# One more pair with seven products, batch 1 transposed in fewer steps, and GpSimd's copy moved up: a fused attention, FFT and FFN kernel on one core

## The chip, the core and the metric

The kernel runs on one core of a Trainium2 chip. A core has TensorE (matrix products, into PSUM), VectorE, ScalarE, GpSimd and SyncE, which here only starts DMAs. In the profile they are PE (and PEld, the weight load), DVE, ACT, POOL and SP. Each runs its own list of instructions in order and meets the others through semaphores. The metric is the device time of one execution in microseconds.

## What is computed

Two batches, 768 rows, 512 columns. Attention in buckets gives x; then a two-dimensional Fourier transform (its real part), a normalised feed-forward network with a hidden width of 2048, and a gated output. The change touches the feed-forward network alone.

```python
def _moe_ref(x, w_ch1, w_ch2) -> np.ndarray:
    X = np.fft.fft(x, axis=1)
    X = np.fft.fft(X, axis=2)
    mixed = np.real(X).astype(np.float32)
    u = x + mixed
    mu = np.mean(u, axis=-1, keepdims=True)
    var = np.mean((u - mu) ** 2, axis=-1, keepdims=True)
    un = (u - mu) / np.sqrt(var + 1e-06)
    ch = np.maximum(un @ w_ch1, 0.0) @ w_ch2
    return (u + ch).astype(np.float32)

def _moe2_ref(x, w_val, conv_w, w_out) -> np.ndarray:
    B, S, D = x.shape
    K = conv_w.shape[0]
    xp = np.concatenate([np.zeros((B, K - 1, D), dtype=np.float32), x], axis=1)
    gate_pre = np.zeros((B, S, D), dtype=np.float32)
    for k in range(K):
        gate_pre += conv_w[k][None, None, :] * xp[:, k:k + S, :]
    gate = 1.0 / (1.0 + np.exp(-gate_pre))
    val = x @ w_val
    return (gate * val @ w_out).astype(np.float32)
```

## The kernel before

Every large product is made of three: each operand is split in a rounded high part (`_hi`, by ScalarE) and the rest (`_lo`, by VectorE or GpSimd), and hi x hi, lo x hi and hi x lo are added in PSUM.

The hidden width is 16 blocks of 128 for each batch, so 32 blocks in all. They are worked in two ways.

**Plain blocks** (`PLAIN` = 8 of batch 0). In step n TensorE does the first half of block n (`ffn1`: 24 matmuls from un to the hidden block, in two chunks of 512 and 256 columns in banks 6 and 7), then the second half of block n - 1 (`ffn2`: four pieces d of 6 matmuls into the accumulators). ScalarE takes the relu (`h_hi`), VectorE the rest (`h_lo`, `relu_lo`), which frees the bank. In `ffn2` of block n, before its piece d = 1, stands `transpose_un(T + n)`: tile n of batch 1 (T = 6 tiles of 128 rows) through bank 6, for n = 0 to 5; it waits until the first chunk of the next block has left bank 6. ScalarE and VectorE then make the tile's high part (`unT_hi`) and low part (`unT_lo`).

**Windows** (`WINDOWS` = 12, each one pair of blocks): the first half of a pair is done with seven products of half size instead of eight (Strassen's scheme), 42 matmuls of 384 columns, each product followed by one piece of the second half of the pair before it; an eighth piece closes the window. The operands of the products are sums: of w1, by GpSimd (`sum_w1_pair`, four additions, and `split_w1_pair`, seven low parts), and of un, by VectorE (`sum_un`, eight additions of 128x768 elements for each batch, and `split_unsum`, four low parts; ScalarE rounds in between with `round_unsum`). For batch 0 these are placed in plain steps 2 to 6; for batch 1 in windows 0 to 3. ScalarE copies the first product of a window out of PSUM (`copy_first`), and VectorE adds the others to it (`add_partial`); TensorE's third product waits for the first such sum.

**The seam** is window `SEAM` = 4, where batch 0 ends and batch 1 begins. In it the accumulators of batch 0 are completed; ScalarE and VectorE copy them out as x2 (`take_x2`), and GpSimd copies four columns at the border of each half for the convolution (`finish_x2`, L755), once all of x2 is there. VectorE (L1554) and ScalarE (L1144) both wait at the end of this window for that copy (`x2_lead` = 2). GpSimd's order in a window is: four low parts of the next pair's w1, low part of w2, the three other low parts of w1, four sums for the pair after that, low part of the other w2; in the seam `finish_x2` follows. Seven windows follow the seam, in which ScalarE and VectorE also do the convolution of batch 0 (`first_tap`, `conv_tap`).

SyncE starts the loads of weights in the order of their use. The load of the first pair of w1 (`load_w1_pair(0)`) waits for the end of the feature transform, since it goes to a place that the transform's tables share; it stands behind the loads of block 3.

## Time and profile before

| what | us |
|---|---|
| median of three runs | 625.12 (624.51 to 625.20) |
| the profiled execution | 624.13 |
| its span, first to last instruction | 622.5 |
| TensorE busy in it | 606.5 |
| VectorE, ScalarE, GpSimd busy | 427.0, 345.5, 342.0 |
| mean granted TensorE clock | 0.997 of full speed |

The plain steps run from about 282 to 346 us of the span, the windows from there to about 549, the output stage to the end. A row of a timeline gives start, duration, engine, line, operation, the tiles it writes and reads, and in brackets the idle time before it with what ended it. Durations of matmuls are longer than the distance of their starts, because they are pipelined: the distance of starts is what counts. The share of busy time is an average over stages; the waits and the stretches tell where an edit can act.

### The profile page before, as it was taken

How to read it: one execution, taken by the hardware profiler on the slowest of the kernel's cores; microseconds unless marked ns; L12 is line 12 of the kernel's file. 1: busy time of each engine (PE TensorE's matmuls, PEld its weight loads, DVE VectorE, ACT ScalarE, POOL GpSimd, SP SyncE). 2: the span in 40 equal slices, each digit the busy share in tenths (PEclk: the TensorE clock that was granted, in tenths of full speed). 3: DMA queues.
4: the chain of work that ended last, by engine and by line, in shares of the span. 5: the costliest groups of instructions: out<-in, count | busy, mean ns of one | idle time of the engine just before them, and what ended most of it. 6: DMA issues, size and time to landing. Idle time of an engine off the chain costs nothing.

```text
span 622.5 us, 10883 instructions
## 1 busy us (share of the span) xinstructions
PE 606.5 (97%) x3682; PEld 503.9 (81%) x3682; DVE 427.0 (69%) x683; ACT 345.5 (55%) x694; POOL 342.0 (55%) x328
## 2 busy tenths in 40 slices
PE   6899999999999999999999999997999999999997
PEld 3677777677777776998888999997899999988886
DVE  3978888888888875887465566635477666569920
ACT  4877777777777784464344444423444444274232
POOL 4543433333347664346335898865699999224140
PEclk9999999999999999999999999999899999999999
DMA  6942323323333020000312122230222222100102
GB/s 139 240 113 64 90 65 89 89 63 90 81 99 98 13 65 1 0 2 6 115 51 67 52 70 68 67 101 19 68 84 84 82 73 66 34 0 1 68 34 103
DMA packets 28178, 42.22 MB, mean 68 GB/s; under 512 B 3440, under 2 KB 16240, under 8 KB 28144
## 3 DMA queue, kind: packets, MB, share of 16 engines
q1 hardware_dynamic: 26176, 37.38, 21.1%
q0 software_dynamic: 1728, 4.02, 2.6%
q10 hardware_dynamic: 240, 0.39, 0.4%
q8 instruction: 18, 0.29, 0.2%
q14 instruction: 16, 0.13, 0.1%
HBM read 38.63 MB, written 3.15 MB: 67 GB/s over the span
## 4 chain that ended last, share of the span: by engine, by line
PE 93%; POOL 2%; DVE 2%; DMA 1%; issue 1%; ACT 1%; SPq 0%; ACTq 0%; DVEq 0%; POOLq 0%
PE banks L1876 21%; PE banks L1908 14%; PE banks L1663 12%; PE banks L1680 11%; PE banks L1730 10%; PE banks L1867 5%; PE banks L1990 5%; PE banks L2006 5%; PE banks L1703 2%; PE banks L1813 2%; PE banks L1616 2%; PE banks L1738 1%; DMA q_raw<-in_q 1%; PE banks L1622 1%; PE banks L1787 1%
## 5 line engine op out<-in xcount | busy, mean ns | idle before, releaser
L1242 DVE TENSOR_REDUCE row_min<-banks 128x1 f32<-128x768 f32 x96 | 91.8, 956 | 32.2 <-PE banks L1663 31.4
L872 ACT ACTIVATE prob<-banks,row_min 128x768 f32<-128x768 f32 x96 | 87.0, 906 | 29.0 <-DVE row_min L1242 28.9
L1730 PE MATMUL banks<-ident,prob 128*128 128x128 f32 x576 | 79.3, 273 | 1.4 <-ACT probT L374 1.4
L1502 DVE TENSOR_TENSOR partial_sums<-banks,partial_sums 128x384 f32<-128x384 f32 x72 | 40.1, 557 | 54.5 <-PE banks L1908 48.7
L1730 PEld LDWEIGHTS banks<-ident,prob 128*128 128x128 f32 x576 | 68.1, 140 | 6.8 <-issue 1.9
L1680 PE MATMUL banks<-probT,v_in 128*64 128x384 f32 x384 | 69.0, 494 | 0.0
L605 POOL TENSOR_TENSOR k_b<-k_raw,k_a 64x768 fp32r<-64x768 f32 x16 | 29.2, 1826 | 70.4 <-ACT k_a L855 70.3
L1876 PE MATMUL banks<-h_hi,w_hi 128*128 128x512 f32 (+1 forms) x256 | 66.4, 341 | 0.0
L1876 PE MATMUL banks<-h_hi,w_lo 128*128 128x512 f32 (+1 forms) x256 | 66.0, 339 | 0.0
L1876 PE MATMUL banks<-h_lo,w_hi 128*128 128x512 f32 (+1 forms) x256 | 65.7, 338 | 0.0
L374 ACT COPY probT<-banks 128x384 f32<-128x384 f32 x104 | 49.0, 479 | 22.5 <-PE banks L1730 22.2
L1663 PE MATMUL banks<-k_a,q_a 128*128 128x384 f32 x192 | 57.2, 379 | 2.6 <-POOL q_a L610 1.8
L1460 DVE SCALAR_TENSOR_TENSOR x_then_u_then_gate<-x2T,taps,x_then_u_then_gate 128x384 f32<-128x384 f32 x64 | 54.9, 862 | 3.9 <-ACT x_then_u_then_gate L1051 2.9
L1509 DVE SCALAR_TENSOR_TENSOR h_lo<-partial_sums,h_hi 128x384 fp32r<-128x384 f32 x48 | 43.0, 916 | 19.7 <-ACT h_hi L1098 19.7
L610 POOL TENSOR_TENSOR q_a<-q_raw,q_a 64x768 fp32r<-64x768 f32 x16 | 29.2, 1824 | 47.7 <-ACT q_a L859 47.5
L1663 PEld LDWEIGHTS banks<-k_a,q_a 128*128 128x128 f32 x192 | 29.5, 189 | 31.4 <-issue 28.5
L676 POOL TENSOR_TENSOR w_lo<-w_stage,w_hi 128x512 fp32r<-128x512 f32 x32 | 43.0, 1345 | 20.0 <-ACT w_hi L908 20.0
L374 DVE COPY probT<-banks 128x384 f32<-128x384 f32 x88 | 48.2, 548 | 2.8 <-PE banks L1730 2.8
L1663 PE MATMUL banks<-k_b,q_b 128*128 128x384 f32 x192 | 49.4, 338 | 0.0
L1680 PEld LDWEIGHTS banks<-probT,v_in 128*64 128x64 f32 x384 | 24.7, 136 | 28.6 <-issue 28.6
L1876 PEld LDWEIGHTS banks<-h_hi,w_hi 128*128 128x128 f32 x256 | 44.0, 189 | 1.5
L1876 PEld LDWEIGHTS banks<-h_lo,w_hi 128*128 128x128 f32 x256 | 39.4, 189 | 5.7
(216 smaller groups left out, 1497.4 us busy)
## 6 DMA issues: line engine op xcount, KB each, us to landing
w_stage<-in_moe_w_ch SPq DMA_DIRECT2D x40, 256.0 KB, 2.7
q_raw<-in_q SPq DMA_DIRECT2D x32, 192.0 KB, 3.3
k_raw<-in_k SPq DMA_DIRECT2D x30, 192.0 KB, 3.6
v_in<-in_v SPq DMA_DIRECT2D x16, 192.0 KB, 2.8
w_pair<-in_moe_w_ch SPq DMA_DIRECT2D x6, 512.0 KB, 3.8
w_stage<-in_moe_w_ch SPq DMA_DIRECT2D x6, 512.0 KB, 3.8
out<-y_out SPq DMA_DIRECT2D x11, 256.0 KB, 2.0
seq_tables_sb<-in_dft POOLq DMA_DIRECT2D x6, 386.0 KB, 3.5
```

The source lines that it names most:

```text
L374: copy(dst, src).then_inc(scratch_free[bank_of(i, use)], 1)
L676: pool.tensor_tensor(w2_lo[:, slot, :], w2_stage[:, slot, :], w2_hi[:, slot, :].bitcast(F32), ALU.subtract).then_inc(w2_lo_done, 1)
L872: act.activation(prob[s % 2][:, :, :], s_tile(s), ACT.Exp, bias=row_min[:, s:s + 1], scale=-1.0, accum_out=row_sum[:, s:s + 1]).then_inc(e ...
L1242: dve.tensor_reduce(row_min[:, s:s + 1], s_tile(s), AX.XY, ALU.min).then_inc(min_ready, 1)
L1460: dve.scalar_tensor_tensor(out=dst, in0=src, scalar=weight, in1=dst, op0=ALU.mult, op1=ALU.add).then_inc(conv_step, 1)
L1502: dve.tensor_tensor(out, product_bank[PRODUCT_BANK[o]], other, ALU.add).then_inc(done, 1)
L1509: dve.scalar_tensor_tensor(out=h_lo[:, slot, cols], in0=quarter[q], scalar=0.0, in1=h_hi[:, slot, cols].bitcast(F32), op0=ALU.max, op1=ALU ...
L1663: op = pe.matmul(s_tile(s)[:, c, :], lhs[:, rows], rhs[:, c * HALF:(c + 1) * HALF], start=start, stop=not start)
L1680: op = pe.matmul(PS[g * D:(g + 1) * D, 7, 0:HALF], v_in[:, h, kt, :], probT[h][:, kt, g * HALF:(g + 1) * HALF], start=(kt == 0), stop=(kt ...
L1730: op = pe.transpose(bank[:, j * P:(j + 1) * P], prob[tile % 2][:, c, j * P:(j + 1) * P], ident[:, :])
L1876: op = pe.matmul(acc(d, c), w_[:, m % 2 if isinstance(m, int) else 1 - slot, cols], h_[:, slot, at:at + size], start=False, stop=last, ski ...
L1908: op = pe.matmul(product_bank[PRODUCT_BANK[o]], w_[:, k, :], x_[:, k, :], start=OPENS_BANK[o] and k == 0 and n == 0, stop=(k == 1 and n == 2),
```

## The change

`PLAIN` goes from 8 to 6, so there are 13 windows instead of 12, five of them ahead of the seam (now window 5). The eight windows from the seam on stay. The six tiles of batch 1 are transposed in four steps: one in each of the second halves of blocks 0 and 1, two in each of blocks 2 and 3. The second tile of such a pair goes through bank 7 and waits for the second chunk's bank; the first half of the block after it waits for the first tile's low part with its first chunk and for the second tile's with its second chunk.

The sums for batch 0 move up with it: VectorE's additions to steps 1, 2 and 3, its low parts to steps 3 and 4, ScalarE's roundings to steps 2, 3 and 4. SyncE's load of the first pair moves ahead of the loads of block 3. In the seam GpSimd's `finish_x2(0)` goes up its order, and ScalarE's three waits at the end of the seam window go to the window behind it, ahead of the first tap. In the rows of the order below, `h_lo` is the low part of a hidden block, `unT1_lo` that of a tile of batch 1, `x_then_u_then_gate` holds VectorE's sums.

VectorE, steps 3 and 4 before:

```order
L1373 SCALAR_TENSOR_TENSOR h_lo<-banks,h_hi 128x512
L1373 SCALAR_TENSOR_TENSOR h_lo<-banks,h_hi 128x256
L1342 TENSOR_TENSOR unT1_lo<-banks,unT1_hi 128x4x128
L1485 TENSOR_TENSOR x_then_u_then_gate<-unT0_hi,unT0_lo 128x768
L1489 TENSOR_TENSOR x_then_u_then_gate<-x_then_u_then_gate 128x768 x2
L1373 SCALAR_TENSOR_TENSOR h_lo<-banks,h_hi 128x512
L1373 SCALAR_TENSOR_TENSOR h_lo<-banks,h_hi 128x256
L1342 TENSOR_TENSOR unT1_lo<-banks,unT1_hi 128x4x128
L1485 TENSOR_TENSOR x_then_u_then_gate<-unT0_hi,unT0_lo 128x768
L1489 TENSOR_TENSOR x_then_u_then_gate<-x_then_u_then_gate 128x768
```

VectorE, steps 3 and 4 now, and the low parts of the last plain block behind them:

```order
L1377 SCALAR_TENSOR_TENSOR h_lo<-banks,h_hi 128x512
L1377 SCALAR_TENSOR_TENSOR h_lo<-banks,h_hi 128x256
L1346 TENSOR_TENSOR unT1_lo<-banks,unT1_hi 128x4x128 x2
L1489 TENSOR_TENSOR x_then_u_then_gate<-unT0_hi,unT0_lo 128x768
L1493 TENSOR_TENSOR x_then_u_then_gate<-x_then_u_then_gate 128x768
L1500 TENSOR_TENSOR unT0_sums_lo<-x_then_u_then_gate,unT0_sums_hi 128x768
L1377 SCALAR_TENSOR_TENSOR h_lo<-banks,h_hi 128x512
L1377 SCALAR_TENSOR_TENSOR h_lo<-banks,h_hi 128x256
L1346 TENSOR_TENSOR unT1_lo<-banks,unT1_hi 128x4x128 x2
L1500 TENSOR_TENSOR unT0_sums_lo<-x_then_u_then_gate,unT0_sums_hi 128x768 x3
L1377 SCALAR_TENSOR_TENSOR h_lo<-banks,h_hi 128x512
```

Each of these two steps now has two tiles, and the four low parts of the sums stand ahead of the hidden blocks' low parts of steps 4 and 5.

GpSimd, the second part of the seam window before:

```order
L785 TENSOR_TENSOR w1_lo<-w1_stage,w1_hi 128x256
L676 TENSOR_TENSOR w2_lo<-w2_stage,w2_hi 128x512
L785 TENSOR_TENSOR w1_lo<-w1_sums,w1_hi 128x256
L785 TENSOR_TENSOR w1_lo<-w1_stage,w1_hi 128x256
L785 TENSOR_TENSOR w1_lo<-w1_sums,w1_hi 128x256
L771 TENSOR_TENSOR w1_sums<-w1_pair_1 128x256
L774 TENSOR_TENSOR w1_sums<-w1_sums,w1_pair_1 128x256
L776 TENSOR_TENSOR w1_sums<-w1_pair_1 128x256
L779 TENSOR_TENSOR w1_sums<-w1_pair_1,w1_sums 128x256
L676 TENSOR_TENSOR w2_lo<-w2_stage,w2_hi 128x512
L755 COPY x2T_0<-x2T_0 128x4x4
```

GpSimd, the same part now:

```order
L786 TENSOR_TENSOR w1_lo<-w1_pair_1,w1_hi 128x256
L677 TENSOR_TENSOR w2_lo<-w2_stage,w2_hi 128x512
L756 COPY x2T_0<-x2T_0 128x4x4
L786 TENSOR_TENSOR w1_lo<-w1_sums,w1_hi 128x256
L786 TENSOR_TENSOR w1_lo<-w1_pair_1,w1_hi 128x256
L786 TENSOR_TENSOR w1_lo<-w1_sums,w1_hi 128x256
L772 TENSOR_TENSOR w1_sums<-w1_stage 128x256
L775 TENSOR_TENSOR w1_sums<-w1_sums,w1_stage 128x256
```

The copy (L755, now L756) stands directly behind the first w2 low part; eight instructions that stood ahead of it stand behind it.

```diff
         def un_bank(n):
-            return [1, 2, 3, 2, 3, 2][n] if n < T else 6
+            return [1, 2, 3, 2, 3, 2][n] if n < T else [6, 6, 6, 7, 6, 7][n - T]
...
-        PLAIN = FB // 2
+        PLAIN = 6
+        TILES_BY = {0: (0,), 1: (1,), 2: (2, 3), 3: (4, 5)}
...
             for n in range(2, PLAIN):
                 load_w(n, n, n % 2)
-                if n == 3:
+                if n == 2:
                     load_w1_pair(0)
...
                 split_w2(PLAIN + 2 * g, 0)
+                if g == SEAM:
+                    finish_x2(0)
                 if more:
                     for o in range(4, 7):
                         split_w1_pair(g + 1, o)
                 if g + 2 < WINDOWS:
                     sum_w1_pair(g + 2)
                 split_w2(PLAIN + 2 * g + 1, 1)
-                if g == SEAM:
-                    finish_x2(0)
...
                 copy_first(g)
                 if more:
                     round_w1_pair(g + 1, 0)
+                if g == SEAM + 1:
+                    act.wait_ge(taps_spread, 2)
+                    act.wait_ge(x2_lead, 2)
+                    act.wait_ge(unsum_lo_done, 8)
                 if g > SEAM:
                     first_tap(0, g - SEAM - 1)
...
-                if g == SEAM:
-                    act.wait_ge(taps_spread, 2)
-                    act.wait_ge(x2_lead, 2)
-                    act.wait_ge(unsum_lo_done, 8)
...
                 relu(n, n % 2)
-                if n <= T:
-                    unT_hi(T + n - 1)
+                tiles = TILES_BY.get(n - 1, ())
+                if tiles:
+                    unT_hi(T + tiles[0])
                 if n < LAG + 1:
                     normalise(T + n + 2)
+                if len(tiles) > 1:
+                    unT_hi(T + tiles[1])
...
-                for i in {4: (0, 1), 5: (2, 3)}.get(n, ()):
+                for i in {2: (0,), 3: (1, 2), 4: (3,)}.get(n, ()):
                     round_unsum(0, i)
...
                 relu_lo(n, n % 2)
-                if n <= T:
-                    unT_lo(T + n - 1)
-                for k in {2: range(3), 3: range(3, 6), 4: range(6, 8)}.get(n, ()):
+                for tile in TILES_BY.get(n - 1, ()):
+                    unT_lo(T + tile)
+                for k in {1: range(3), 2: range(3, 6), 3: range(6, 8)}.get(n, ()):
                     sum_un(0, k)
-                for i in {5: (0, 1), 6: (2, 3)}.get(n, ()):
+                for i in {3: (0,), 4: (1, 2, 3)}.get(n, ()):
                     split_unsum(0, i)
...
                 if n >= T:
-                    pe.wait_ge(h_lo_done, 2 * (n - T + 1) + 1)
+                    by = next(m for m in TILES_BY if n - T in TILES_BY[m])
+                    pe.wait_ge(h_lo_done, 2 * (by + 1) + 1 + TILES_BY[by].index(n - T))
...
-                    if c == 0 and isinstance(n, int) and 2 <= n <= T + 1:
-                        pe.wait_ge(unT_lo_done, T + n - 1)
+                    tiles = TILES_BY.get(n - 2, ()) if isinstance(n, int) else ()
+                    if c < len(tiles):
+                        pe.wait_ge(unT_lo_done, T + tiles[c] + 1)
...
                 for d in range(KB):
-                    if d == 1 and n < T:
-                        transpose_un(T + n)
+                    if 0 < d <= len(TILES_BY.get(n, ())):
+                        transpose_un(T + TILES_BY[n][d - 1])
                     second(n, slot, d, False)
```

## Rows read from the trace of the kernel before

**Rows 1.** The page, part 1: busy us, share of the span, instructions.

```profile
PE 606.5 (97%) x3682; PEld 503.9 (81%) x3682; DVE 427.0 (69%) x683; ACT 345.5 (55%) x694; POOL 342.0 (55%) x328
```

**Rows 2.** Who waited for whom, 340 to 620 us: total, times, longest.

```profile
PE banks L1908 <- DVE partial_sums L1502: 4.4, 1, 4.4
```

**Rows 3.** Busy time by stretch: length, five engines, clock, DMA share, GB/s.

```profile
428.08:450.12 22.04, 17.61 (x94) 16.15 (x92) 9.79 (x15) 7.10 (x16) 15.77 (x19) 0.92 0.18 60
450.12:465.88 15.76, 15.76 (x93) 14.74 (x92) 11.59 (x14) 7.89 (x17) 15.68 (x16) 1.00 0.25 83
```

**Rows 4.** Timeline of TensorE, first window behind the seam: start, duration, instruction.

```profile
432.01 0.51 PE L1876 MATMUL banks<-h_lo,w_hi 128*128 128x512 f32 x2
436.95 0.45 PE L1908 MATMUL banks<-unT_sums_hi,w_first_hi 128*128 128x384 f32 x1 [4.43 <-DVE partial_sums L1502]
...
437.76 0.52 PE L1908 MATMUL banks<-unT_sums_hi,w_first_lo 128*128 128x384 f32 x1
...
441.23 0.34 PE L1908 MATMUL banks<-unT_sums_hi,w_hi 128*128 128x384 f32 x1
```

**Rows 5.** Timeline of GpSimd, second part of the seam window.

```profile
428.09 1.06 POOL L785 TENSOR_TENSOR w_lo<-w_sums,w_hi 128x256 fp32r<-128x256 f32 x1
...
431.32 0.74 POOL L771 TENSOR_TENSOR w_sums<-w_pair 128x256 f32<-128x256 f32 x1
...
434.18 1.26 POOL L676 TENSOR_TENSOR w_lo<-w_stage,w_hi 128x512 fp32r<-128x512 f32 x1
435.39 0.20 POOL L755 COPY x2T<-x2T 128x16 f32<-128x16 f32 x1
```

**Rows 6.** Timelines of VectorE and ScalarE at the seam.

```profile
424.86 0.42 DVE L1473 COPY x2T<-banks 128x256 f32<-128x256 f32 x1
...
427.46 3.12 DVE L1509 SCALAR_TENSOR_TENSOR h_lo<-partial_sums,h_hi 128x384 fp32r<-128x384 f32 x3 [0.47 <-ACT h_hi L1098]
436.34 0.56 DVE L1502 TENSOR_TENSOR partial_sums<-banks,partial_sums 128x384 f32<-128x384 f32 x1 [5.76 <-ACT partial_sums L1091]
...
428.78 0.61 ACT L908 CAST w_hi<-w_stage 128x512 fp32r<-128x512 f32 x1
435.66 0.48 ACT L1091 COPY partial_sums<-banks 128x384 f32<-128x384 f32 x1 [6.28 <-POOL x2T L755]
```

**Rows 7.** Timeline of TensorE, one plain step.

```profile
315.58 0.39 PE L1867 MATMUL banks<-unT_hi,w_hi 128*128 128x512 f32 x1
...
319.79 0.52 PE L1876 MATMUL banks<-h_hi,w_hi 128*128 128x512 f32 x2
...
320.85 0.60 PE L1787 MATMUL banks<-ident,un 128*128 128x128 f32 x4
...
324.45 0.39 PE L1867 MATMUL banks<-unT_hi,w_hi 128*128 128x512 f32 x1
```

**Rows 8.** Timelines of VectorE and GpSimd: two operations together, and one alone.

```profile
331.59 2.06 DVE L1496 TENSOR_TENSOR unT_sums_lo<-x_then_u_then_gate,unT_sums_hi 128x768 fp32r<-128x768 f32 x1
...
331.54 1.30 POOL L671 TENSOR_TENSOR w_lo<-w_stage,w_hi 128x512 fp32r<-128x512 f32 x1 [4.62 <-ACT w_hi L903]
...
313.84 0.95 DVE L1485 TENSOR_TENSOR x_then_u_then_gate<-unT_hi,unT_lo 128x768 f32<-128x768 f32 x1
```

**Rows 9.** Timelines of ScalarE and VectorE in the same plain step.

```profile
321.49 0.59 ACT L953 CAST unT_hi<-banks 128x512 fp32r<-128x512 f32 x1 [1.11 <-PE banks L1787]
...
319.20 0.69 DVE L1373 SCALAR_TENSOR_TENSOR h_lo<-banks,h_hi 128x512 fp32r<-128x512 f32 x1 [0.48 <-ACT h_hi L985]
...
322.11 0.69 DVE L1342 TENSOR_TENSOR unT_lo<-banks,unT_hi 128x512 fp32r<-128x512 f32 x1 [1.27 <-ACT unT_hi L953]
```

**Rows 10.** Loads (the page, part 6), end of the feature transform, rounding of w1 (timelines).

```profile
w_pair<-in_moe_w_ch SPq DMA_DIRECT2D x6, 512.0 KB, 3.8
...
281.59 0.28 PE L1813 MATMUL banks<-feat_sin_lo_sb,y_hi 128*128 128x256 f32 x1
...
296.07 0.60 ACT L903 CAST w_hi<-w_stage 128x512 fp32r<-128x512 f32 x1
```

## The prediction

> **What bounds the kernel now.** The page's busy line first: TensorE works 606.5 of 622.5 us [rows 1], and the chain that ended last is TensorE's almost throughout, so an edit pays only if it takes time or a wait out of TensorE's own queue. So the list of who waited for whom, over the feed-forward stage, is read for TensorE: one wait stands out, 4.4 us on VectorE's partial_sums [rows 2]. Its releasers on the other timelines: VectorE had waited 5.76 us for ScalarE's copy of the first product, ScalarE 6.28 us for GpSimd's x2T copy (L755) [rows 6]. Those three are one stall. Third, the stretches: an ordinary window takes 15.76 us; the first window after the seam takes 22.04, with 17.61 us of TensorE busy and a mean granted clock of 0.92 [rows 3]. That is 6.28 us too much. TensorE's timeline splits it: the last matmuls of the second product's step are issued at 432.01, the next is at 436.95 (4.43 us idle), and from 437.76 to 441.23 a 384-column matmul starts every 0.32 us instead of 0.175 [rows 4]. That is the lower of the two clock levels, 1.2 against 2.4 GHz, granted after the idle stretch; 3.47 us of it cost about 1.7.
>
> Cause of the stall: GpSimd's copy of four columns starts at 435.39. Ahead of it in GpSimd's order stand three w1 splits from 428.09, four sums from 431.32 and the w2 split of 434.18, eight instructions and 7.3 us, of which none is an input of the copy [rows 5]. Its inputs are x2 pieces, VectorE's last at 424.86 plus 0.42. ScalarE had done its own queue at 428.78 + 0.61 = 429.39 and VectorE at 430.58 [rows 6]; both then sat in the waits that end their seam window (L1144, L1554), with the first product's copy behind ScalarE's, and TensorE's third product behind that.
>
> **The change, part by part.**
>
> *The copy moved up and ScalarE's wait moved back.* GpSimd now comes to the copy behind the first w2 split of the seam, at 428.09 on the old clock [rows 5], 2.8 us after its inputs are there; it takes 0.20, so done at 428.3. VectorE's wait at the window's end (430.58) is then met. ScalarE no longer waits there: it goes on at 429.39 to the copy of the first product, ready at about the same time, and holds its wait before the first tap, where it is also already met. Then what is late next? VectorE's first sum needs ScalarE's copy (0.48 us, so 429.9) and the second product (about 431.4), and with its 0.56 us it ends near 432.0 [rows 6]; TensorE would start the third product at 432.35. It isn't late, as in each ordinary window, which has the same steps and no idle. GpSimd's eight instructions come 0.2 us later: its w2 split ends at 435.7 and TensorE wants it at 428.08 + 9.5 = 437.6, 9 pieces of 1.05 into the window. ScalarE's next two roundings need GpSimd's second and third sum, about 432.9 and 433.5 by 0.74 us each, about 1.8 us later than ScalarE could take them, but their users come a whole window later. So the window falls to 15.76: **-6.28 us**. Ends: all of it, or nothing if another input holds the copy.
>
> *One pair more with seven products.* TensorE's plain step, as the timeline shows it: first half of a block 315.58 to 319.79, 4.21 us; second half of the block before it to 324.45, 4.66, of which the transposition takes about 0.44 (four matmuls and the restart behind them), so 4.22; together 8.43 [rows 7]. Two blocks are 16.86 us, a window 15.76. **-1.10 us.** The six transpositions of batch 1 stay six, only two steps carry two each: 0. The stages behind keep their counts (eight windows from the seam on).
>
> *The preparation squeezed into fewer blocks.* VectorE's eight sums and four low parts for batch 0 now follow in steps 1 to 4 instead of 2 to 6, ahead of the low part of the next hidden block, for which TensorE waits (before a transposition, because the bank is shared, and at the first window). How long are they? Alone 0.95 us; beside a GpSimd instruction 2.06: VectorE's began at 331.59, GpSimd's at 331.54 ran 1.30, and VectorE's ended 0.8 after it [rows 8]. So I let the two engines alternate: each VectorE operation costs 0.95 plus the rest of GpSimd's one.
> Step 3: TensorE's transpositions stand at 311.98 (320.85 less a period of 8.87) and 0.44 + 1.05 later, at 313.47. ScalarE takes a tile 0.64 after, VectorE 0.62 after that, in 0.69 [rows 7, 9]: free at 315.42. GpSimd then has one 128x512 split (1.25) and sums of 0.7 without a pause, so three operations end at 315.42 + 3 x 0.95 + 1.1 + 0.7 + 0.7 = 320.8. The first low part of step 4, which ScalarE allows from 319.2 + 0.44, takes 0.6 more: 321.45. TensorE wants it before that step's transposition, at 320.85 + 0.44 = 321.29: with the semaphore **+0.25 us**.
> Step 4: second tile at 321.54 + 1.49, low part done at 324.98, three operations against three GpSimd splits of 0.7: 329.9 at the latest, 329.5 if the first meets little; plus 0.6. TensorE is ready for the first window at 319.79 + 0.44 + 8.87 + 0.44 + 0.25 = 329.79. **+0.5 us.**
> Step 1: the sums start when TensorE has ended block 0, at 297.84 (315.58 less two periods); only one GpSimd operation meets them: 297.9 + 2.9 + 1.25 = 302.1, the low part done at 302.7, wanted at 303.1: 0.
> Bounds: with 0.95 for each operation no wait at all; with 2.06 for each of three in steps 1, 3 and 4 waits of about 1.8, 0.9 and 2.2: 0 to 4.9 us. I take 0.75, since it goes by the alternation that the rows of both engines show.
> The Trainium skill ("SBUF — State Buffer", section "SBUF: two separate sides") says the same of this pair: a VectorE operation with two SBUF inputs and a GpSimd operation that reads SBUF take a shared port pair by an exclusive lock, and the later one blocks until the first is done. It speaks against this change. By it the sum is the one made here; had these operations not met, it would be 0.75 us lower. The trace agrees (0.95 against 2.06 us).
>
> *Loads.* The load of the first pair now stands ahead of w1 of block 3 in SyncE's queue and waits for the end of the feature transform (about 282 [rows 10]). Behind it w1 of block 3 starts there instead of before; a load lands in 3.8 us at most, so by about 287, and ScalarE takes this block at 296.07 [rows 10]: 0. If that cover were gone, it would cost the 3.8.
>
> *Sum.* 624.13 of the profiled execution (span 622.5 and 1.6 around it) - 6.28 - 1.10 + 0.75 = 617.5. The median of the runs stands 1.0 above the profiled execution, at 625.12, so **618.5 us** for it.
>
> **Rivals.**
> A. *The stall shrinks only in part.* For: the stall has three links, and the trace shows only which came last. Against: each other input has a row 2 us or more ahead. If TensorE kept half of the wait, and with it part of the low clock, the gain would be 3 + 0.35: 621.8. If the copy moved nothing, 624.8 with the squeeze.
> B. *VectorE is later in the plain blocks than alternation says*, because an operation loses the port twice. Price: up to 4.9 instead of 0.75, so 622.6; middle 620.5. For: steps 3 and 4 have no slack. Against: 2.06 is the longest of the kind, and it met one of GpSimd's longer instructions.
> C. *Slower.* The mechanism is the clock: the 4.43 us idle was followed by 3.47 us at the low level, together 6.1. If VectorE's lateness in steps 3 and 4 became two stalls of that kind, it would cost 12.2 and give 625.1 - 7.4 + 12.2 = 629.9. It decides from waits of over 8.6 us with what the clock adds. Against: my upper bound is 4.9 in three pieces, the largest 2.2.
> D. *No change within 0.2%*: the copy isn't freed and the squeeze costs what the pair saves; 624.8.
>
> **How the numbers follow.** Forecast 0.79 (own range 617.2 to 620), A with a part kept 0.06, B 0.09, C 0.03, D 0.03. About 0.2%, 1.2 us, is what a measurement of this kernel can tell from no change. Faster 0.94, same 0.03, slower 0.03. Range: low end the sum without any new wait, 617.7, less 0.6 for the spread of the runs; high end to B's middle and a bit: 617.1 to 620.9.
>
> **What would show it.** Profile of the changed kernel: the window behind the seam at 15.8 us, granted clock 1.00, no wait of ScalarE for x2T over 1 us; the copy 0.2 us after the seam's first w2 split; five windows before the seam of 15.76 each; TensorE idle for a few tenths before the first transposition of step 4 and before the first window, with VectorE's h_lo or unT_sums_lo as releaser; VectorE's sums in these steps alternating with GpSimd. Wrong would be: a stall behind the seam with another releaser, over 1.5 us at the first window, or a low clock in the plain blocks.

## The result: 616.67 us against 625.07

| kernel | median of the runs | profiled execution | its span | mean granted clock |
|---|---|---|---|---|
| before | 625.07 (4 runs, 624.51 to 625.20) | 624.13 | 622.5 | 0.997 |
| changed | 616.67 (4 runs, 616.41 to 617.67) | 616.41 | 614.7 | 1.000 |

The ratio is 0.987, with a 95% interval of 0.9853 to 0.9887. The forecast was 618.5 in a range of 617.1 to 620.9: its sign and its chief term are right, its number is 1.8 us too high, and the time lies 0.4 us below the range. Measured a second time, the changed kernel gave 616.51 (4 runs, 0.9862 [0.9845, 0.9878]).

### The profile page after: what moved, and what is told of

Same layout as the page of the kernel before. It is cut to its first block, busy times and chain, and to the rows that moved or that the text cites. A ratio compares the mean times of both kernels' runs of the same rounds, so it can differ in the third digit from the quotient of the medians.

```text
span 614.7 us, 10917 instructions
## 1 busy us (share of the span) xinstructions
PE 605.4 (98%) x3676; PEld 503.5 (82%) x3676; DVE 431.1 (70%) x689; ACT 347.6 (57%) x700; POOL 349.3 (57%) x337
## 4 chain that ended last, share of the span: by engine, by line
PE 95%; DVE 2%; DMA 1%; ACT 1%; POOL 1%; issue 0%; ACTq 0%; POOLq 0%
PE banks L1882 22%; PE banks L1914 16%; PE banks L1667 12%; PE banks L1684 11%; PE banks L1734 10%; PE banks L1996 5%; PE banks L2012 5%; PE banks L1873 4%; PE banks L1707 2%; PE banks L1818 2%; PE banks L1620 2%; DMA k_raw<-in_k 1%; PE banks L1742 1%; PE banks L1858 1%; PE banks L1626 1%; PE banks L1792 1%
## 5 line engine op out<-in xcount | busy, mean ns | idle before, releaser
L1506 DVE TENSOR_TENSOR partial_sums<-banks,partial_sums 128x384 f32<-128x384 f32 x78 | 43.4, 557 | 54.9 <-PE banks L1914 54.7
L1513 DVE SCALAR_TENSOR_TENSOR h_lo<-partial_sums,h_hi 128x384 fp32r<-128x384 f32 x52 | 46.4, 912 | 21.5 <-ACT h_hi L1099 21.5
L1099 ACT ACTIVATE h_hi<-partial_sums 128x384 fp32r<-128x384 f32 x52 | 25.9, 521 | 38.1 <-PE banks L1882 36.1
```

The source lines that it names most:

```text
L1506: dve.tensor_tensor(out, product_bank[PRODUCT_BANK[o]], other, ALU.add).then_inc(done, 1)
L1513: dve.scalar_tensor_tensor(out=h_lo[:, slot, cols], in0=quarter[q], scalar=0.0, in1=h_hi[:, slot, cols].bitcast(F32), op0=ALU.max, op1=ALU ...
```

## The profile after

The busy line of the changed kernel, and its clock in 40 slices (compare [rows 1]; the one 8 in the clock row of before is gone):

```profile
PE 605.4 (98%) x3676; PEld 503.5 (82%) x3676; DVE 431.1 (70%) x689; ACT 347.6 (57%) x700; POOL 349.3 (57%) x337
PEclk9999999999999999999999999999999999999999
```

Stretches of the changed kernel: the first window, the window behind the seam, and the one after it. Columns as in [rows 3]: length, busy time of each engine with instructions, granted clock, share of the DMA engines, GB/s.

```profile
330.07:345.80 15.73, 15.73 (x89) 14.70 (x90) 9.43 (x12) 6.24 (x16) 14.78 (x18) 1.00 0.24 67
427.27:443.07 15.80, 15.80 (x94) 14.77 (x92) 10.11 (x15) 7.22 (x16) 15.43 (x19) 1.00 0.29 84
443.07:458.77 15.70, 15.70 (x92) 14.67 (x91) 11.53 (x14) 7.89 (x17) 15.62 (x16) 1.00 0.27 84
```

The window behind the seam is now a window like the others: 15.80 us, TensorE busy all through, full clock, where [rows 3] had 22.04 at 0.92. The list of waits, read for TensorE from 290 to 560 us, is empty; [rows 2] had 4.4 us there.

The seam on GpSimd, ScalarE, VectorE and TensorE in that order (compare [rows 4 to 6]):

```profile
425.96 1.36 POOL L677 TENSOR_TENSOR w_lo<-w_stage,w_hi 128x512 fp32r<-128x512 f32 x1 [0.19 <-ACT w_hi L909]
427.26 0.53 POOL L756 COPY x2T<-x2T 128x16 f32<-128x16 f32 x1
427.75 1.09 POOL L786 TENSOR_TENSOR w_lo<-w_sums,w_hi 128x256 fp32r<-128x256 f32 x1
...
428.60 0.48 ACT L1092 COPY partial_sums<-banks 128x384 f32<-128x384 f32 x1
432.52 0.41 ACT L1087 CAST w_first_hi<-w_sums 128x256 fp32r<-128x256 f32 x1 [2.53 <-POOL w_sums L775]
...
430.81 0.56 DVE L1506 TENSOR_TENSOR partial_sums<-banks,partial_sums 128x384 f32<-128x384 f32 x1 [1.55 <-PE banks L1914]
...
431.21 0.51 PE L1882 MATMUL banks<-h_lo,w_hi 128*128 128x512 f32 x2
431.56 0.34 PE L1914 MATMUL banks<-unT_sums_hi,w_first_hi 128*128 128x384 f32 x1
```

The copy of four columns starts at 427.26, directly behind the first w2 low part. ScalarE copies the first product at 428.60; in [rows 6] it did so at 435.66. VectorE's first sum, at 430.81, now waits for TensorE and not the other way round, and the third product at 431.56 has no bracket: it follows the matmul ahead of it.

**Where 8.8 us went.** The profiled execution of before is from the fast end of its runs, as will be shown. Before was profiled twice more, and the third profile, of 625.20 us and close to the median, serves here. Its window behind the seam, its last copy and store, and the same of the changed kernel:

```profile
428.13:450.83 22.70, 18.29 (x94) 16.83 (x92) 9.78 (x15) 7.09 (x16) 15.74 (x19) 0.85 0.20 58
...
619.90 0.37 ACT L1197 COPY y_out<-banks 128x256 f32<-128x256 f32 x1 [1.01 <-PE banks L2020]
620.30 0.33 SPq L575 DMA_DIRECT2D out<-y_out  x1
```

```profile
612.14 0.37 ACT L1201 COPY y_out<-banks 128x256 f32<-128x256 f32 x1 [1.01 <-PE banks L2026]
612.54 0.33 SPq L576 DMA_DIRECT2D out<-y_out  x1
```

| stretch | before, third profile | changed | difference |
|---|---|---|---|
| to the opening of the feed-forward accumulators, behind the first half of block 0 (L1853, now L1858) | 286.55 | 286.79 | +0.24 |
| from there to the window behind the seam | 141.58 | 140.48 | -1.10 |
| the window behind the seam | 22.70 | 15.80 | -6.90 |
| from there to ScalarE's last copy | 169.07 | 169.07 | 0 |
| from that copy to the end of the span | 3.60 | 2.56 | -1.04 |

The sum is -8.80, and the two times differ by 8.79. The medians differ by 8.40: the changed kernel's median is 0.26 above its profiled execution, and that of before 0.13 below this one.

## Experiments

Three questions. First, is it the copy's place, ScalarE's wait, or the pair that pays? Second, is the stall set by GpSimd's order instruction by instruction, and does the low clock follow the length of the wait? Third, why is the squeeze of VectorE's work free, and how near is it to costing something?

**1. The two edits at the seam alone** (eight plain blocks kept).

```diff
                 split_w2(PLAIN + 2 * g, 0)
+                if g == SEAM:
+                    finish_x2(0)
...
                 split_w2(PLAIN + 2 * g + 1, 1)
-                if g == SEAM:
-                    finish_x2(0)
...
+                if g == SEAM + 1:
+                    act.wait_ge(taps_spread, 2)
+                    act.wait_ge(x2_lead, 2)
+                    act.wait_ge(unsum_lo_done, 8)
                 if g > SEAM:
                     first_tap(0, g - SEAM - 1)
...
-                if g == SEAM:
-                    act.wait_ge(taps_spread, 2)
-                    act.wait_ge(x2_lead, 2)
-                    act.wait_ge(unsum_lo_done, 8)
```

> Kernel before (8 plain blocks, 12 windows) with the two edits of the seam alone: GpSimd's copy behind the first w2 low part, ScalarE's three waits in the window behind. Theory (two parts that add, no cost in the plain steps): the window behind the seam falls from 22.04 to 15.76 us, so 6.3 us less, 618.8. Rival (part of the 8.4 us gain comes from how the parts meet, or from the end of the program): more than 7.0 less here, under 618.1, or under 6 less. Last matmul to the end of the span: 3.3 us as before if it belongs to the kernel's layout, about 2.6 if it varies.

617.38 us (5 runs), 0.989 [0.9874, 0.9905]. The window behind the seam:

```profile
427.98:443.75 15.77, 15.77 (x93) 14.74 (x92) 9.98 (x15) 7.22 (x16) 15.40 (x19) 1.00 0.27 84
```

The whole stall is gone with the seam edits alone. The median fell 7.75 us against 625.13 of the runs of before beside it, 1.4 us more than was expected; measured against the third profile of before, the window loses 22.70 - 15.77 = 6.93 of that, and the rest is in the tail (below). So the rival of this expectation, a part of the gain at the end of the program, came true beside the theory.

**2. The pair and the squeeze alone** (the changed kernel with both seam edits undone).

```diff
-                if g == SEAM:
-                    finish_x2(0)
...
                 split_w2(PLAIN + 2 * g + 1, 1)
+                if g == SEAM:
+                    finish_x2(0)
...
-                if g == SEAM + 1:
-                    act.wait_ge(taps_spread, 2)
-                    act.wait_ge(x2_lead, 2)
-                    act.wait_ge(unsum_lo_done, 8)
                 if g > SEAM:
                     first_tap(0, g - SEAM - 1)
...
+                if g == SEAM:
+                    act.wait_ge(taps_spread, 2)
+                    act.wait_ge(x2_lead, 2)
+                    act.wait_ge(unsum_lo_done, 8)
```

> Changed kernel with the seam as before: 6 plain blocks, 13 windows, tiles in pairs, but GpSimd's copy last and ScalarE's waits at the end of the seam window. Theory: 1.10 us less than before, 624.0, with the stall of 4.4 us and the low clock behind the seam as before. The recorded prediction's cost of the squeeze (0.75 us) would give 624.7. Rival of an extra gain in this part: 623 or less.

623.28 us (7 runs), 0.9972 [0.9961, 0.9983]. The stall is there as before (22.47 us, clock 0.85, a wait of 4.45), and the plain part has gained its pair:

```profile
428.09:450.56 22.47, 18.02 (x94) 16.56 (x93) 9.79 (x15) 7.10 (x16) 15.78 (x19) 0.85 0.19 59
```

The accumulators were opened 1.07 later than in the third profile of before (287.62 against 286.55), and the window behind the seam begins at nearly the same time, 428.09 against 428.13: the plain part and its five windows took 140.47 us instead of 141.58. That is -1.1 us without a squeeze to pay for, and the median is 0.7 us below what was expected; the tail is 1.0 us shorter here too (below).

**3. The copy alone**, ScalarE's waits left at the end of the window.

```diff
                 split_w2(PLAIN + 2 * g, 0)
+                if g == SEAM:
+                    finish_x2(0)
...
                 split_w2(PLAIN + 2 * g + 1, 1)
-                if g == SEAM:
-                    finish_x2(0)
```

> Kernel before with GpSimd's copy moved alone; ScalarE keeps its wait at the end of the seam window. Theory: the copy lands near 428.3, before ScalarE gets there at 429.4, so the moved wait is worth nothing and the time is that of the seam alone, 618.8. Rival (both edits are needed): a stall of 1 us or more stays, 620 or more.

**4. ScalarE's waits alone**, the copy left at the end of GpSimd's order.

```diff
+                if g == SEAM + 1:
+                    act.wait_ge(taps_spread, 2)
+                    act.wait_ge(x2_lead, 2)
+                    act.wait_ge(unsum_lo_done, 8)
                 if g > SEAM:
                     first_tap(0, g - SEAM - 1)
...
-                if g == SEAM:
-                    act.wait_ge(taps_spread, 2)
-                    act.wait_ge(x2_lead, 2)
-                    act.wait_ge(unsum_lo_done, 8)
```

> Kernel before with ScalarE's waits moved alone; the copy stays last in GpSimd's order. Theory: ScalarE copies the first product at 429.4, but VectorE still waits for the copy until 435.6 at the end of its window and adds the second product only then: TensorE's wait shrinks by ScalarE's 0.5 us at most, with the low clock behind it, 624.3 to 625.1. Rival (ScalarE's wait is the link that counts): 619 to 621.

The copy alone: 618.20 us (4 runs), 0.9896 [0.9881, 0.9911]. The waits alone: 623.83 us (11 runs), 0.9978 [0.9969, 0.9987]. The first is 0.6 us below its expectation, the second 0.5 below the lower end of its own. The window behind the seam with the copy alone, and ScalarE's copy of the first product in it:

```profile
428.77:444.54 15.77, 15.77 (x94) 14.75 (x92) 9.98 (x15) 7.21 (x16) 15.40 (x19) 1.00 0.26 84
...
430.18 0.48 ACT L1091 COPY partial_sums<-banks 128x384 f32<-128x384 f32 x1
```

With the waits alone, the window, and ScalarE, VectorE and TensorE at the same place:

```profile
428.32:450.78 22.46, 18.67 (x94) 17.20 (x93) 9.78 (x15) 7.20 (x16) 15.72 (x19) 0.85 0.21 59
...
429.65 0.48 ACT L1091 COPY partial_sums<-banks 128x384 f32<-128x384 f32 x1
...
435.92 0.56 DVE L1502 TENSOR_TENSOR partial_sums<-banks,partial_sums 128x384 f32<-128x384 f32 x1 [5.10 <-POOL x2T L755]
...
436.53 0.69 PE L1908 MATMUL banks<-unT_sums_hi,w_first_hi 128*128 128x384 f32 x1 [3.79 <-DVE partial_sums L1502]
```

The copy's place removes the stall alone; ScalarE's waits are worth nothing beside it in the window (15.77 with and without them moved). Moved alone they let ScalarE go at 429.65, but VectorE stays in its own wait for the copy, 5.10 us, and TensorE waits 3.79 instead of 4.4. This is what a wait with two holders looks like: the first releaser that the timeline names, ScalarE, was only one of two engines that stood before the same door.

**The tail.** Of the 1.3 us by which the fourth kernel's median is below before, the window gives little (22.46 against 22.70 of the third profile). Most is in the tail. SyncE's last wait, for the last store to land, stands in the list of waits as line, releaser, total, times, longest. For before (third profile) and the changed kernel:

```profile
SPq L577 <- DMA out<-y_out: 2.4, 1, 2.4
```

```profile
SPq L578 <- DMA out<-y_out: 1.4, 1, 1.4
```

It was 1.9 with the copy alone and 1.4 with the waits alone. The DMA packets show what lies between. From 1.8 us after ScalarE's last copy begins to the end of the span, before (third profile) has ten packets and the changed kernel has none:

```profile
DMA packets 10, 0.02 MB, mean 9 GB/s; under 512 B 1, under 2 KB 9, under 8 KB 9
q1 hardware_dynamic: 9, 0.01, 1.7%
q14 instruction: 1, 0.01, 1.1%
```

```profile
DMA packets 0, 0.00 MB, mean 0 GB/s; under 512 B 0, under 2 KB 0, under 8 KB 0
```

The store is 128 packets of 1 KB. In before 120 of them are done at 1.7 us after the copy begins, and the last eight come one after another from 2.26 on (the ninth packet of q1 is the 4 bytes that close it). They start in the moment at which a packet of 8 KB ends, of the kind that the profile calls `instruction` (by its name a load of program code): it ran from 1.96 to 2.26.

**5 to 7. The copy at three places between.** The same one edit, with the copy ahead of GpSimd's last w2 low part (5), between the second and the third of the four sums (6), or ahead of the four sums (7), and ScalarE's waits where they were.

```diff
                 if g + 2 < WINDOWS:
                     sum_w1_pair(g + 2)
+                if g == SEAM:
+                    finish_x2(0)
                 split_w2(PLAIN + 2 * g + 1, 1)
-                if g == SEAM:
-                    finish_x2(0)
```

That is kernel 5; in kernel 7 the two added lines stand ahead of `if g + 2 < WINDOWS:`, and in kernel 6 inside `sum_w1_pair`, ahead of its third addition, for the call from the seam.

> Kernel before with GpSimd's copy one instruction up, ahead of the last w2 low part of the seam (1.2 us earlier). TensorE's wait behind the seam: 3.2 us instead of 4.4. Theory (the low clock is a second cost of the idle stretch, all or nothing, and differs from run to run in length): a low spell is still there, time 1.2 us less, 623.9, mean granted clock of the runs still near 0.994 to 0.997. Rival (the low clock costs in proportion to the wait): 1.2 + a quarter of 1.7 to 2.7 less, 623.2 to 623.4.

> Kernel before with GpSimd's copy between the second and third of the four sums (2.5 us earlier). TensorE's wait: 1.9 us. Theory all or nothing: if no low spell follows so short an idle stretch, the whole of the clock's cost goes too and only 1.9 us of the gain of the seam is missing: 619.3, mean clock 1.0. Rival in proportion: 1.9 + 0.43 of the clock's 1.7 to 2.7 missing, 620.0 to 620.5.

> Kernel before with GpSimd's copy directly ahead of the four sums (4.0 us earlier). Both theories: TensorE waits 0.3 to 0.5 us, no low spell, 617.7 to 618.3, 0.4 above the seam alone (617.4).

The window behind the seam and TensorE's third product in each, in the order 5, 6, 7:

```profile
427.83:448.63 20.80, 17.58 (x94) 16.18 (x93) 9.99 (x15) 7.09 (x16) 15.86 (x19) 0.92 0.20 64
...
435.48 0.69 PE L1908 MATMUL banks<-unT_sums_hi,w_first_hi 128*128 128x384 f32 x1 [3.22 <-DVE partial_sums L1502]
```

```profile
428.06:447.51 19.45, 17.62 (x94) 16.17 (x92) 10.61 (x15) 7.09 (x16) 15.73 (x19) 0.91 0.20 68
...
434.34 0.45 PE L1908 MATMUL banks<-unT_sums_hi,w_first_hi 128*128 128x384 f32 x1 [1.83 <-DVE partial_sums L1502]
```

```profile
428.90:445.14 16.24, 16.07 (x94) 14.77 (x92) 11.47 (x15) 7.21 (x16) 15.57 (x19) 1.00 0.27 82
...
433.50 0.45 PE L1908 MATMUL banks<-unT_sums_hi,w_first_hi 128*128 128x384 f32 x1 [0.17 <-DVE partial_sums L1502]
```

The fourth column is the window less the 15.76 us of an ordinary one and less the wait; where the window's clock is under 1.00 that is what the low clock cost.

| copy stands | TensorE's wait | window behind the seam | over 15.76, less the wait | median |
|---|---|---|---|---|
| last (before: three profiles) | 4.4 | 22.04, 22.01, 22.70 | 1.85, 1.83, 2.53 | 625.07 |
| ahead of the last w2 low part (5) | 3.22 | 20.80 | 1.82 | 623.98 (10 runs), 0.9986 [0.9974, 0.9999] |
| after two of four sums (6) | 1.83 | 19.45 | 1.86 | 621.93 (5 runs), 0.9947 [0.993, 0.9965] |
| ahead of the sums (7) | 0.17 | 16.24 | 0.31, clock 1.00 | 619.0 (4 runs), 0.9902 [0.9885, 0.9919] |
| behind the first w2 low part (3) | 0 | 15.77 | 0 | 618.20 (4 runs) |

The wait falls as the instructions that no longer stand ahead of the copy would have it: 1.2 us for a w2 low part, 1.4 for two sums, 1.7 for the next two. So the length of the stall is set by GpSimd's order, instruction by instruction. The price of the clock does not fall with it. A wait of 1.83 us was followed by as much low clock (1.86 us of cost) as one of 4.43 had been; one of 0.17 us was followed by none. Kernel 5 was expected at 623.9 and took 623.98. Kernel 6 was expected at 619.3 if no low clock follows so short a gap (the theory), and at 620 to 620.5 if its price shrinks with the wait (the rival); both were too low. Kernel 7 took 619.0, 0.7 over the upper end of its expectation, with 0.48 us more in the window than an ordinary one. A part of both misses is the base: they were counted from kernel 1 (617.4), which has the short tail, and kernels 6 and 7 have the long one. From kernel 3, with the long tail, the sums are 618.20 + 1.83 + 1.86 = 621.9 for kernel 6, as measured, and 618.7 for kernel 7.

Nor is the clock's price the same each time. Of kernel 6's five runs four had a mean clock of 0.997 and 621.6 to 622.4 us, and one had 1.000 and 620.38. No trace stands behind that one, but its clock says that the low spell was absent, and it is about 1.6 us below the median of the five.

**8 and 9. VectorE made later.** The changed kernel, with one (9) or two (8) more subtractions of 128x768 elements in step 4 ahead of the last plain block's low part. They write to a place that is written again later, so they are work added, with a wait of VectorE for each to end.

```diff
                 for i in {3: (0,), 4: (1, 2, 3)}.get(n, ()):
                     split_unsum(0, i)
+                if n == 4:
+                    for again in range(1):
+                        dve.tensor_tensor(unsum_lo[1][:, again, :, :], unsum[:, 3, :, :],
+                                          unsum_hi[0][:, 3, :, :].bitcast(F32), ALU.subtract).then_inc(again_done, 1)
+                        dve.wait_ge(again_done, again + 1)
```

> Changed kernel with one more 128x768 subtraction by VectorE at the end of step 4, behind the four low parts and ahead of the low part of the last plain block. Theory (the squeeze costs nothing because VectorE is done just in time, with 0.2 to 0.4 us to spare before the first window): TensorE waits 0.6 to 1.2 us ahead of the first window. Rival (VectorE has room to spare in these steps): no wait.

> The same with two more subtractions. Theory: TensorE waits 1.6 to 2.6 us ahead of the first window, one operation of 0.95 to 1.4 us more than with one, and possibly a low spell behind it as with the 1.83 us wait at the seam. Rival: under 1 us.

One more operation: 618.41 us (one run). GpSimd's low part that it met, the operation, TensorE's first product, and the first window:

```profile
328.39 2.00 POOL L678 TENSOR_TENSOR w_lo<-w_stage,w_hi 128x512 fp32r<-128x512 f32 x1
...
329.16 2.03 DVE L1571 TENSOR_TENSOR unT_sums_lo<-x_then_u_then_gate,unT_sums_hi 128x768 fp32r<-128x768 f32 x1
...
332.07 0.41 PE L1920 MATMUL banks<-unT_hi,w_first_hi 128*128 128x384 f32 x1 [1.90 <-DVE h_lo L1378]
```

```profile
332.07:347.93 15.86, 15.86 (x91) 14.80 (x91) 8.35 (x12) 4.79 (x11) 14.25 (x16) 1.00 0.19 60
```

Two more: 620.7 us (one run), with a wait of 3.29 and a low spell in the window behind it:

```profile
332.82 0.41 PE L1920 MATMUL banks<-unT_hi,w_first_hi 128*128 128x384 f32 x1 [3.29 <-DVE h_lo L1378]
```

```profile
332.82:350.21 17.39, 17.39 (x91) 16.19 (x91) 7.87 (x12) 4.79 (x11) 13.78 (x15) 0.90 0.13 45
```

From the opening of the accumulators to the first window the changed kernel takes 43.28 us (286.79 to 330.07); with one more operation, of 2.03 us, it takes 45.07, and with two, of 3.43 together, 46.47. So 0.24 us of the added work is free in both: that is VectorE's slack at this place, and 0.19 of it is its wait for ScalarE in the changed kernel (rows below). The second operation lengthened the wait by 1.39 us and brought the clock's cost with it, 17.39 - 15.73 = 1.66. Both waits are longer than expected, since the added operation met a GpSimd instruction of 2.00 us. And a wait of 1.90 us had no low clock behind it, where at the seam one of 1.83 had. Kernel 9's mean clock of 0.997 comes from the start of the program, where 10 to 20 us have 0.84.

**10 to 12. The same kernels again.** Before twice more and the changed kernel once more, with no edit, to see how much of a single profile is its own.

> The kernel before once more, for a second profiled execution. Theory (the recorded profile had a short low spell, clock 0.997 against 0.994 in most timed runs, and that is why the seam's cost was read too small): a profiled execution with clock 0.994 shows TensorE's wait at 4.4 us again and a low spell of 5 to 8 us instead of 3.5, and the window behind the seam at 23 to 24 us instead of 22.0. Rival (the missing microsecond is somewhere else, at the start or at the end of the program): the window at 22.0 again, with clock 0.997, and other places longer.

> The kernel before a third time for its trace. Both profiled executions so far had a clock of 0.996 to 0.997 and 624.1 us, while the median of the timed ones has 0.994 and 625.1. Theory: with 0.994 the first accumulators open at 287.2 to 287.6 instead of 286.5 (a low spell at the start of the program, as in the copy-alone run), or the window behind the seam takes 22.5 or more; the rest of the span is the same. Rival: the difference lies in another place.

> The changed kernel once more. Theory: 616.4 to 617.7, clock 1.000 in most runs and 0.997 in some, window behind the seam 15.8 in each; last matmul to the end of the span 2.6 to 3.3 us as in the others.

Before again: 625.3 us (10 runs), 1.0006 [0.9993, 1.002], so two equal kernels do read as equal; its profiled execution fell at 624.07, clock 0.996. The third profile is of an execution of 625.20 us, clock 0.994. Its window of 22.70 is as expected of it (22.5 or more); the 23 to 24 us that the earlier expectation gave for a clock of 0.994 did not come. The changed kernel again took 616.51 us (4 runs, 615.88 to 616.71), as expected. The window behind the seam in the second profile of before, TensorE's restart in the third, and the changed kernel's window again:

```profile
428.18:450.19 22.01, 17.59 (x94) 16.19 (x92) 9.79 (x15) 7.10 (x16) 15.75 (x19) 0.92 0.21 60
```

```profile
436.98 0.69 PE L1908 MATMUL banks<-unT_sums_hi,w_first_hi 128*128 128x384 f32 x1 [4.41 <-DVE partial_sums L1502]
...
441.94 0.34 PE L1908 MATMUL banks<-unT_sums_hi,w_hi 128*128 128x384 f32 x1
```

```profile
426.71:442.51 15.80, 15.80 (x94) 14.77 (x92) 10.13 (x15) 7.23 (x16) 15.44 (x19) 1.00 0.26 84
```

In the third profile the matmuls are slow from the restart at 436.98 to 441.94, 4.96 us; in the profile on which the prediction rests they ran at full speed for 0.8 us after the restart and then slow for 3.47 [rows 4]. The wait ahead is the same in both, 4.41 and 4.43. So the window is 22.04 or 22.70 by how long the low level (1.2 of 2.4 GHz) lasts. Of the 20 runs of before that stand beside kernels 5, 6, 7 and 10, the eight with a mean clock of 0.996 or 0.997 took 624.1 to 624.8 us, the nine with 0.994 or 0.995 took 624.8 to 625.7, and the three with 0.989 or 0.992 took 626.3 to 626.7. So the time of before goes with its mean clock, and the first profile is from the fast end. A mean clock does not say where the low level was, though: runs of the changed kernel, which has no stall, have 0.997 too (four of its eight).

## The prediction, step by step

The forecast was 1.83 us too high. Three steps of it failed: the end of the program, put at nothing (1.04); the low clock behind the stall, too small by 0.62; and the cost of the squeeze (0.75), which did not come. Against them stand 0.24 of a later start, 0.27 between the changed kernel's profile and its median, and 0.07 by which the third profile of before stands above 624.13 + 1.0.

**The bound and the cause: right.** TensorE's queue was the bound, three links made one stall, and the copy's place in GpSimd's order was its cause. Kernels 5 to 7 and 3 show it: moved by one, three, five and eight instructions, the copy takes the wait from 4.4 to 3.2, 1.8, 0.2 and 0. Its inputs were there when the trace had said. Rival A (another input holds the stall) and D (nothing moves) did not occur.

**The seam, -6.28: the mechanism right, the size 0.6 too small.** The term was read from one execution with 1.7 us of low clock. In the four profiles where the wait of about 4.4 us was left (before three times, kernel 2), the window lost 1.83, 1.85, 2.26 and 2.53 to the clock. The execution near the median had 22.70, so the edit took out 6.90. The first profile's own number could have warned: its execution stood 1.0 below the median.

**"The median of the runs stands 1.0 above the profiled execution", +1.0: wrong for the changed kernel.** This is in the main the miss above seen from the other side, not a further one. The distance was treated as a property of the measurement and carried over. Between the first and the third profile of before, 0.66 us of it is the longer window (22.70 against 22.04) and 0.29 the longer tail (3.60 against 3.31). The changed kernel has neither, and its median stands 0.26 above its profile, 0.63 the second time. Without the +1.0 the sum is 617.5, 0.8 from the result, but with errors that partly cancel: it would start 1.07 too low and still lack the tail.

**The pair, -1.10: right to the hundredth.** From the opening of the accumulators to the window behind the seam 141.58 us became 140.48, in its second profile 140.46, and with the pair alone 140.47.

**The squeeze, +0.75: not there.** TensorE has no wait in the plain steps. The rows of steps 3 and 4 on VectorE, and GpSimd beside step 3, in the changed kernel:

```profile
315.61 2.06 DVE L1489 TENSOR_TENSOR x_then_u_then_gate<-unT_hi,unT_lo 128x768 f32<-128x768 f32 x1
317.71 1.38 DVE L1493 TENSOR_TENSOR x_then_u_then_gate<-x_then_u_then_gate 128x768 f32<-128x768 f32 x1
319.01 1.50 DVE L1500 TENSOR_TENSOR unT_sums_lo<-x_then_u_then_gate,unT_sums_hi 128x768 fp32r<-128x768 f32 x1
320.43 1.11 DVE L1377 SCALAR_TENSOR_TENSOR h_lo<-banks,h_hi 128x512 fp32r<-128x512 f32 x2
324.92 4.12 DVE L1500 TENSOR_TENSOR unT_sums_lo<-x_then_u_then_gate,unT_sums_hi 128x768 fp32r<-128x768 f32 x3
329.23 0.69 DVE L1377 SCALAR_TENSOR_TENSOR h_lo<-banks,h_hi 128x512 fp32r<-128x512 f32 x1 [0.19 <-ACT h_hi L986]
...
315.56 1.30 POOL L672 TENSOR_TENSOR w_lo<-w_stage,w_hi 128x512 fp32r<-128x512 f32 x1 [6.26 <-ACT w_hi L904]
316.82 1.46 POOL L772 TENSOR_TENSOR w_sums<-w_pair 128x256 f32<-128x256 f32 x1
318.35 1.34 POOL L775 TENSOR_TENSOR w_sums<-w_sums,w_pair 128x256 f32<-128x256 f32 x1
...
321.57 0.60 PE L1792 MATMUL banks<-ident,un 128*128 128x128 f32 x4
330.07 0.41 PE L1914 MATMUL banks<-unT_hi,w_first_hi 128*128 128x384 f32 x1
```

The two engines do take turns: the first operation took 2.06 beside GpSimd's of 1.30, just as the row of before. But the next ones took 1.38 and 1.50, where the working gave each 0.95 + 0.7 = 1.65, and in step 4 three took 4.12, 1.37 each. An operation that waits pays 0.43 to 0.55 us for a 128x256 instruction of GpSimd (0.7 alone), not the whole of it. The row of before had this already: there the operation paid 1.11 for one of 1.30. The working took that 1.1 for the first operation but the whole 0.7 for the others. The three ended at 320.5, which is 320.2 on the clock of before (there the accumulators open 0.28 earlier, 286.51), instead of 320.8; the low part in front of the transposition started at 320.43, both of its step were done by 321.54, and TensorE's transposition stands at 321.57 with no wait. In step 4 the three ended at 329.04, so 328.8 against 329.5 to 329.9 in the working, and then VectorE even waited 0.19 us for ScalarE. The term's structure is right (kernels 8 and 9: beyond 0.24 us TensorE waits for every bit of added work), and it was mis-sized by 0.15 to 0.3 us for each operation. It was taken as a sure cost where a slack of two tenths decides between nothing and something; the working was not good to two tenths, and the lower bound, 0, would have been as well founded.

The Trainium skill ("SBUF — State Buffer", section "SBUF: two separate sides") says that such a VectorE operation and a GpSimd instruction hold the port pair one at a time. The trace agrees in 2.06 us against 0.95 alone. The 0.15 to 0.3 us by which each turn came out shorter than the two instructions one after the other decided the term here.

**The third product not late, ScalarE's roundings and the loads at nothing: right.** VectorE's first sum was ready before it (430.81 + 0.56 against 431.56); ScalarE waited 2.53 us for GpSimd's sum at 432.52, more than the 1.8 expected, and TensorE did not wait for it. (That a load lands in 3.8 us "at most" was a slip: the row gives the median.) **ScalarE's moved wait** was told as part of the seam's cure; kernel 3 shows that in the window it does nothing once the copy is early.

**The tail, put at nothing by leaving it out of the sum: -1.04.** From ScalarE's last copy to the end of the span, 3.60 us became 2.56. The work is the same: the store starts 0.40 after the copy in each. It lands sooner: SyncE waits 1.4 us for it, in before 1.9 to 2.4. All fourteen profiles fall into two groups: 1.9 to 2.4 in the three of before and in kernels 3, 5, 6 and 7, and 1.4 in the two of the changed kernel and in kernels 1, 2, 4, 8 and 9. In each of the first seven an `instruction` packet of 8 KB is under way in the middle of the store, and the store's last eight packets start when it ends, to within 0.01 us: at 1.98, 1.99, 2.01, 2.02, 2.11, 2.24 and 2.26 us after the last copy begins. In each of the other seven no such packet falls there, and the store is done at 1.7. In kernels 1 and 4 it comes at 3.5 and 3.8, after the store, and in those with six plain blocks it came 17 us before the end of the span. So the edits moved this load out of the store's way: moved waits of ScalarE (kernels 1 and 4) or six plain blocks (kernel 2) are enough, and the copy's place (kernels 3, 5, 6, 7) does not do it. That the eight packets wait for that load is read from the times; no run here moves it by itself, and why these edits move it is not shown.

**Rivals B and C.** VectorE did not come later than the alternation says but earlier. C would need two stalls; kernel 8 shows its price per stall in this place, 3.29 + 1.66 us, but it took 3.4 us of added work to get there.

Put together: 625.20 + 0.24 - 1.10 - 6.90 - 1.04 = 616.40 for the profiled execution, and 0.27 more to the median.

## To carry to other kernels

Profile the kernel before more than once where its profiled time is not at the median, and ask which part of the profile is short in it; the distance belongs to a term, and may leave with it. When a stall is read, list every engine that waits for its last link: the cure is at the link, and moving one holder of the wait gives almost nothing. A step forecast at a few tenths of a us late should be given as "nothing or a few tenths", and an idle gap of TensorE should be priced with the low clock behind it, since a gap of 1.83 us could draw as much of it as one of 4.4. And look at what the DMA queues carry when the last store runs: a load of a few tenths of a us in its way costs that much of the kernel's time.

## What the runs showed of the hardware

- The low clock level behind an idle gap is neither proportional to the gap nor fixed: behind 4.41 to 4.45 us idle it cost 1.83 to 2.53 us, behind 3.79 us 2.91, behind 3.22 us 1.82, behind 1.83 us 1.86 in the profiled run and by the mean clock nothing in another, behind 1.90 us (at the first window) nothing.
- There is a second place where it comes and goes: in the profiles of kernels 3, 7 and 9 the stretch from 10 to 20 us had a clock of 0.84, 0.83 and 0.84, and the feed-forward accumulators were opened at 287.22, 287.32 and 287.00. In the eleven others the clock there was 1.00, and they were opened at 286.25 to 286.79 in ten, but at 287.62 in kernel 2, so the clock is not all that moves the start. Kernel 3:

```profile
10.00:20.00 10.00, 9.41 (x45) 6.34 (x46) 7.23 (x11) 6.39 (x12) 5.08 (x3) 0.84 0.42 103
```

- GpSimd's copy of 16 elements in each partition, 0.20 us at the end of its order before [rows 5], took 0.53 us in its new place, 0.53 in kernel 3 and 0.19 in kernel 7. It cost nothing here.
- A store came later where a load of instructions fell beside it: the same 128 KB landed 1.4 us after SyncE began to wait where no `instruction` packet ran beside it (seven profiles), and 1.9 to 2.4 us where one of 8 KB did (seven profiles). One sixteenth of the store, eight packets of 1 KB, started as that packet ended.
